# Attention, routed experts and an MLP on one core: the MLP takes the tokens in the order of their experts, and its first weights are prepared among the experts

## What is computed

```python
skip_score = x @ w_skip
do_compute = skip_score > 0
xc = x[do_compute]
logits = xc @ w_gate
e_idx = np.argmax(logits, axis=1)
for e in range(E):                       # 8 experts, hidden size 1024
    mask = e_idx == e
    h = np.maximum(xc[mask] @ w1[e], 0.0)
    y[mask] = gate_w[mask, None] * (h @ w2[e])
out[do_compute] = xc + y                 # the other tokens pass unchanged
...
h = x @ w_in                             # 512 -> 2048
g = h * np.clip(h + 3.0, 0.0, 6.0) / 6.0
return g @ w_out                         # 2048 -> 512
```

## Time and profile before

| | us |
|---|---|
| median of 3 runs (687.64 to 688.62) | 687.93 |
| the profiled execution's own time | 686.13 |
| its span | 684.5 |
| TensorE busy | 643.4 (94%) |
| VectorE busy | 397.9 (58%) |
| ScalarE busy | 323.6 (47%) |
| GpSimd busy | 71.6 (10%) |
| experts, from the first y to the last | 142 to 278.5 |
| MLP, from its first product | 290.4 to 681.2 |

### The profile page before, as it was taken

The page is one execution under the profiler, slowest core; times in us unless marked ns, Lnnn a source line. Parts: engine busy times, 40 slices in busy tenths (PEclk is TensorE's granted clock), DMA queues, the critical chain, the costliest instruction groups (busy, mean ns, idle before and its releaser), DMA issues.

```text
span 684.5 us, 17259 instructions
## 1 busy us (share of the span) xinstructions
PE 643.4 (94%) x6528; PEld 558.1 (82%) x6528; DVE 397.9 (58%) x1043; ACT 323.6 (47%) x675; POOL 71.6 (10%) x122
## 2 busy tenths in 40 slices
PE   5799986789999999989999999999999999999998
PEld 4678875667777887778889889898988988898986
DVE  2568875201111111568777767977777688777753
ACT  3689884011111111465544455655454566454433
POOL 4323452411111111000000000000000000000000
PEclk9999998789999999999999999999999999999999
DMA  9868869788587168632222221532222224212102
GB/s 169 168 161 195 197 180 385 234 304 313 191 274 274 31 216 271 204 101 63 77 78 78 61 71 54 200 118 93 82 63 62 62 68 148 63 61 63 32 0 93
DMA packets 118818, 95.10 MB, mean 139 GB/s; under 512 B 62737, under 2 KB 94485, under 8 KB 118752
## 3 DMA queue, kind: packets, MB, share of 16 engines
q1 hardware_dynamic: 103280, 61.79, 32.3%
q10 hardware_dynamic: 12496, 26.11, 11.2%
q0 software_dynamic: 2976, 6.32, 2.6%
HBM read 80.01 MB, written 17.52 MB: 142 GB/s over the span
## 4 chain that ended last, share of the span: by engine, by line
PE 80%; DMA 7%; DVE 6%; ACT 3%; issue 2%; SPq 1%; another core or an unknown queue 0%; POOLq 0%; POOL 0%; DVEq 0%; ACTq 0%
PE bank L1007 29%; PE av L956 25%; PE av L932 8%; PE bank L920 8%; DMA xin<-x_rows 5%; PE av L777 2%; PE bank L733 2%; DVE sm L1360 2%; PE bank L793 1%; PE bank L718 1%; PE av L889 1%; ACT pr L1054 1%; PE av L944 1%; DVE xall L1373 1%; DMA ot<-x_new 1%
## 5 line engine op out<-in xcount | busy, mean ns | idle before, releaser
L1007 PE MATMUL bank<-o_hi,g_lo 128*128 128x512 f32 x288 | 114.2, 397 | 0.0
L1007 PE MATMUL bank<-o_lo,g_hi 128*128 128x512 f32 x288 | 113.8, 395 | 0.0
L1007 PE MATMUL bank<-o_hi,g_hi 128*128 128x512 f32 x288 | 112.0, 389 | 0.0
L956 PE MATMUL av<-xc_hi,w_hi 128*128 128x384 f32 x342 | 89.1, 341 | 3.7 <-issue 1.9
L956 PE MATMUL av<-xc_hi,w_lo 128*128 128x384 f32 x342 | 87.7, 337 | 0.0
L956 PE MATMUL av<-xc_lo,w_hi 128*128 128x384 f32 x342 | 87.3, 336 | 0.0
L956 PEld LDWEIGHTS av<-xc_hi,w_hi 128*128 128x128 f32 x342 | 62.4, 188 | 19.3 <-DVE act L1615 3.6
L1622 DVE TENSOR_TENSOR g_lo<-act,g_hi 128x384 fp32r<-128x384 f32 x96 | 53.3, 555 | 40.2 <-ACT g_hi L1234 37.1
L920 PEld LDWEIGHTS bank<-xeT,w1s 128*64 128x64 f32 x2176 | 70.1, 140 | 6.5 <-issue 3.8
L920 PE MATMUL bank<-xeT,w1s 128*64 128x64 f32 x2176 | 72.3, 225 | 1.8 <-ACT xeT L1131 0.5
L1234 ACT CAST g_hi<-act 128x384 fp32r<-128x384 f32 x96 | 49.5, 516 | 50.9 <-DVE act L1615 50.9
(11 more groups left out here) (157 smaller groups left out, 910.2 us busy)
## 6 DMA issues: line engine op xcount, KB each, us to landing
w2s<-in_moe_w ACTq DMA_DIRECT2D x7, 2048.0 KB
wor<-in_moe_w_out SPq DMA_DIRECT2D x24, 512.0 KB, 3.7
w1s<-in_moe_w ACTq DMA_DIRECT2D x5, 2048.0 KB, 16.2
wir<-in_moe_w_in SPq DMA_DIRECT2D x24, 256.0 KB, 4.2
wir<-in_moe_w_in SPq DMA_DIRECT2D x48, 128.0 KB, 4.0
qraw<-in_q SPq DMA_DIRECT2D x36, 128.0 KB
vnow<-in_v SPq DMA_DIRECT2D x36, 128.0 KB
x_new<-xall SPq DMA_DIRECT2D x18, 256.0 KB
```

What stands on the lines that cost most here:

```text
L956: last = pe.matmul(into[:, 0:GN], a[it % 2][:, W_AT[w], c, :], b[:, X_AT[x], c, :], start=(n == 0 and fresh), stop=(n == 3 * XQ * len(pair ...
L1007: last = pe.matmul(bank[tile][:, :], a[c][:, i * P:(i + 1) * P], b[it % 2][:, units(it)[c], :], start=(plain(it) and c in (0, 2) and n == ...
```

## The change

The MLP no longer needs the tokens in their own order. `x_rows` gets a region of N + 64 rows ahead of the experts' regions. Skipping tokens count as a ninth class (`NC = NE + 1`), whose rows begin at 0 of that region: they are scattered straight to where the MLP reads them. The results of an expert tile are stored behind them as 64 consecutive rows with two direct DMAs (expert e begins at `first_row[e]`, in `rows_tbl`; rows beyond an expert's count are overwritten by the next expert). `x_new`, its 18 stores from the attention stage and the scatter by half rows are gone. The MLP reads 128 consecutive rows of 520 values; GpSimd copies their token numbers to `tok` (`take_tokens`) and scatters the results to the output by indirect DMA, 128 rows of 512 values each (`store_out`, 18 of them, on GpSimd instead of SP). SP waits before the first six tiles only for the `needed` expert tiles, those of experts that begin below row 768, and for all of them before it loads the second group.

The slices of the MLP's steps 0 and 1 are loaded by SP ahead of the rows of experts 2, 3, 4 and 5, and split by ScalarE behind the tiles of experts 3, 4 and 5 and by VectorE behind those of 3, 4 and 6. Tiles 3 to 5 of the first group get memory of their own (`x_first`). TensorE's spare matmuls between the experts and the MLP are removed.

```diff
+    R0 = N + ET
+    NC = NE + 1
...
-        xn = [put("X", f"xn{i}", [P, DM]) for i in range(3)]
+        xn = [put("X", f"xn{i}", [P, 2, HW]) for i in range(3)]
...
+        sums_at = at["X"]
         xd = [put("X", f"xd{i}", [P, XQ, GN]) for i in range(4)]
+        at["X"] = sums_at
+        x_first = [put("X", f"x_first{i}", [P, 2, HW]) for i in range(3)]
...
-        yo = sb("yo", [P, DH])
+        yo = sb("yo", [P, HW])
...
-        x_rows = nc.dram_tensor("x_rows", [(NE - 1) * R + TMAX * ET + ET, XW], fp32).ap()
-        x_new = nc.dram_tensor("x_new", [N, DM], fp32).ap()
+        x_rows = nc.dram_tensor("x_rows", [R0 + (NE - 1) * R + TMAX * ET + ET, XW], fp32).ap()
...
-            def store_x(T):
-                sp.wait_ge(s_x, T + 1)
-                sp.dma_start(x_new[T * P:(T + 1) * P, :].rearrange("s (h c) -> s h c", h=2), xall[:, T, :, 0:DH]).then_inc(s_xst, 16)
-
...
-            for T in range(1, NT + STORE):
+            for T in range(1, NT):
                 for n in loads_of(T):
                     load_qk(n)
-                if T < NT:
-                    load_v(T)
-                if T >= STORE:
-                    store_x(T - STORE)
-                if T == NT - 1:
-                    load_w1(sp, 0, s_wp1[0])
-                    load_w2(sp, 0, s_wp2[0])
-                    load_w1(sp, 1, s_wp1[1])
+                load_v(T)
+            load_w1(sp, 0, s_wp1[0])
+            load_w2(sp, 0, s_wp2[0])
+            load_w1(sp, 1, s_wp1[1])
...
+            for e, first, end in expert_tiles(sp, first_bounds(sp)):
...
+                elif e == 2:
+                    load_w_in(0)
+                elif e == 3:
+                    load_w_out(0)
+                elif e == 4:
+                    load_w_in(1)
+                elif e == 5:
+                    load_w_out(1)
+                with sp.Fori(0, end - first) as t:
+                    g = first + t
+                    row = t * ET + (R0 + e * R)
+                    sp.wait_ge(s_xet, g + XT0)
+                    sp.wait_ge(s_xmid, g + XM0)
+                    load_rows(bass.ds(row, ET))
+
...
+            total = end
+            sp.wait_ge(s_first, 1)
+            needed = sp.value_load(rows_tbl[0:1, NE:NC], min_val=0, max_val=TMAX)
+            sp.wait_ge(s_xet, total + XT0)
+            sp.wait_ge(s_xmid, total + XM0)
+            load_rows(slice(R0, R0 + ET))
+
...
-                sp.dma_start(x_tile(G, i)[:, :], x_new[T * P:(T + 1) * P, :]).then_inc(x_loaded(G, i)[0], 16)
...
-
-            for it in range(2):
-                load_w_in(it)
-                load_w_out(it)
-            sp.wait_ge(s_xst, 16 * NT)
-            sp.wait_ge(s_yst, total * 16 + YS0)
+                    sp.wait_ge(s_tok, T - 2)
+                sp.dma_start(x_tile(G, i)[:, :, :].rearrange("p h c -> p (h c)"), x_rows[T * P:(T + 1) * P, :]).then_inc(x_loaded(G, i)[0], 16)
+
+            sp.wait_ge(s_yst, needed * 32 + YS0)
...
+                if it == 0:
+                    sp.wait_ge(s_yst, total * 32 + YS0)
...
-            pool.wait_ge(s_xst, 16 * NT)
...
+            pool.wait_ge(s_first, 1)
             for e, first, end in expert_tiles(pool, bounds):
+                base = pool.value_load(rows_tbl[0:1, e:e + 1], min_val=0, max_val=N)
                 with pool.Fori(0, end - first) as t:
+                    row = t * ET + base
                     pool.wait_ge(s_yc, first + t + 1 + YC0)
                     fixed(pool)
-                    pool.indirect_dma_start(out=x_new.rearrange("n (h c) -> (n h) c", h=2),
-                                            out_offset=bass.IndirectOffsetOnAxis(ap=ytok[:, :], axis=0),
-                                            in_=yo[:, :], in_offset=None, bounds_check=2 * N - 1, oob_is_err=False).then_inc(s_yst, 16)
+                    for h in range(2):
+                        pool.dma_start(x_rows[bass.ds(row, ET), h * HW:(h + 1) * HW], yo[h * ET:(h + 1) * ET, :]).then_inc(s_yst, 16)
...
+            def take_tokens(G, i):
+                T = G * MT + i
+                pool.wait_ge(*x_loaded(G, i))
+                pool.tensor_copy(tok[:, T:T + 1], x_tile(G, i)[:, 0, TOKEN:TOKEN + 1]).then_inc(s_tok, 1)
+
+            def store_out(G, i, rows, signal):
+                T = G * MT + i
+                pool.wait_ge(s_tok, T + 1)
+                pool.indirect_dma_start(out=out, out_offset=bass.IndirectOffsetOnAxis(ap=tok[:, T:T + 1], axis=0),
+                                        in_=rows, in_offset=None, bounds_check=N - 1, oob_is_err=False).then_inc(signal, 16)
...
+            for G in range(MG - 1):
+                if G + 2 < MG:
+                    for i in range(3):
+                        take_tokens(G + 2, i)
+                for i in range(MT):
+                    pool.wait_ge(s_oca, MT * G + i + 1)
+                    store_out(G, i, ot[i % 3][:, :], s_ost[i % 3])
...
+            for i in range(3):
+                pool.wait_ge(s_oca, MT * MG - MT + i + 1)
+                store_out(MG - 1, i, ot[i][:, :], s_ost[i])
+            for i in range(3, 5):
+                pool.wait_ge(s_ocd, i - 2)
+                store_out(MG - 1, i, last_out(i), s_last)
+            pool.wait_ge(s_oca, MT * MG - MT + 4)
+            store_out(MG - 1, 5, last_out(5), s_last)
...
-            idle_turns(4)
-            total = tile_bound(pe, NE)
-            pe.wait_ge(s_xetc, total + 1)
-            fixed(pe)
-            idle_turns(3)
             for i in range(MT):
                 transpose_tile(0, i)
+            pe.wait_ge(s_xetc, end + 1)
+            pe.wait_ge(s_yc, end + YC0)
+            fixed(pe)
...
+                if e == 3:
+                    w_high(0)
+                    w_rest_high(0)
+                elif e == 4:
+                    o_high(0)
+                elif e == 5:
+                    w_high(1)
+                    w_rest_high(1)
...
-                sc.copy(xn[i - 3][:, cols], bank[i][:, cols]).then_inc(s_oca, 1)
...
-            total = sc.value_load(tbl[0:1, NE:NE + 1], min_val=1, max_val=TMAX)
-            sc.wait_ge(s_y, total)
-            fixed(sc)
-            w_high(0)
-            w_rest_high(0)
-            w_high(1)
-            w_rest_high(1)
-            o_high(0)
+                sc.wait_ge(s_tok, NT)
+                sc.copy(last_out(i)[:, cols], bank[i][:, cols]).then_inc(s_oca, 1)
...
-            take_last(5, slice(0, DH))
-            take_last(5, slice(DH, DM))
-            sc.wait_ge(s_oca, MT * MG - MT + 5)
-            sc.dma_start(out[N - P:N, DH:DM], xn[2][:, DH:DM]).then_inc(s_last, 16)
+            take_last(5, slice(0, DM))
...
+                then(dve.tensor_scalar(oh[:, 0:GT, NE:NC], skip, 0.0, 0.0, ALU.is_gt, ALU.is_equal))
...
-                then(dve.tensor_scalar(pskip[:, :], skip.rearrange("p t a -> p (t a)"), 0.0, float(NE * R), ALU.is_le, ALU.mult))
...
-                dve.tensor_tensor(pos[:, cols], psel[:, :], pskip[:, :], ALU.add).then_inc(s_pos, 1)
+                dve.tensor_copy(pos[:, cols], psel[:, :]).then_inc(s_pos, 1)
...
+            then(dve.tensor_tensor_scan(routed[:, :], one8[:, :], cnt[:, 0:NE], 0.0, ALU.mult, ALU.add))
+            then(dve.scalar_tensor_tensor(out=first_row[:, 0:NE], in0=routed[:, :], scalar=cnt[:, NE:NC], in1=cnt[:, 0:NE],
+                                          op0=ALU.add, op1=ALU.subtract))
+            then(dve.scalar_tensor_tensor(out=early[:, :], in0=first_row[:, 0:NE], scalar=float(MT * P), in1=ntl1[:, :],
+                                          op0=ALU.is_lt, op1=ALU.mult))
+            then(dve.tensor_reduce(first_row[:, NE:NC], early[:, :], axis=AX.X, op=ALU.add))
+            dve.tensor_copy(rows_tbl[:, :], first_row[:, :]).then_inc(s_first, 1)
...
-                    dve.wait_ge(s_yst, g * 16 + YS0)
-                    dve.tensor_copy(ytok[:, :], xres[:, TOKEN:TOKEN + 1])
+                    dve.wait_ge(s_yst, g * 32 + YS0)
+                    dve.tensor_copy(yo[:, DH:HW], xres[:, DH:HW])
                     dve.wait_ge(s_y, g + 1)
...
+                if e == 3:
+                    w_low(0)
+                elif e == 4:
+                    combine_w(1)
+                    o_low(0)
+                elif e == 6:
+                    w_low(1)
...
+                if G == 0:
+                    dve.wait_ge(s_tok, MT)
```

211 lines of the change are left out of this document (95 added, 116 removed).

## The result

The change made the kernel slower: 694.76 us (median of 5, 693.23 to 698.71) against 687.64 for 5 runs of before, ratio 1.0113 [1.0087, 1.0139]; on another chip 1.0170 [1.0146, 1.0193]. The time lies outside the range forecast (681.0 to 690.0), above it, where a small gain had been forecast. The profiled execution of the changed kernel is the slowest of its five, 698.71, and its span is 697.1.

A forecast was written before the change was run, and what follows sets the result against it. TensorE was taken to bound experts and MLP, with 11.9 us between last y and first product as the seam. Terms -8.0 + 4.4 + 0.8 + 0.2 + 0 = -2.6 us gave a median of 685.3, range 681.0 to 690.0.

The forecast's parts named there:

- The seam, -8.0: Between the experts' last y and the first MLP product: tiles loaded early, first product at 282.4 instead of 290.39, -8.0 us.
- the splits left in place: At the seam: weight splits not moved among the experts would delay the first product until 285.9, by 3.5 us.
- The end, +4.4: Last stores: GpSimd issues six scatters one behind the other, span ends at 688.9 against 684.5, +4.4 us.
- and 0.4 for the end as before: End of the kernel: from the last scatter's landing at 688.5 to the span's end, 0.4 us, giving 688.9.
- its upper bound of +6.4: End of the kernel: +6.4 us at the most, if each scatter's issue takes 1.30 us instead of 0.97.
- GpSimd's token copies at the seam: Seam: six copies of token numbers, due about 6 us after the first product, GpSimd free near 281; cost nothing.
- The experts, +0.8: Expert tiles: weights in SP's queue, results' stores and VectorE's splits move in; between 0 and +10, taken as +0.8 us.
- rival C: Experts: row loads of experts 2 to 5 stuck behind new weights in SP's queue; +10 us, 694.5; chance 0.15.
- Routing and attention, +0.2 and 0 (-2 to +1): Before the experts: ninth class on the chain +0.2 us; added rows against removed stores 0, bounds -2 and +1.
- the sign that it is wrong altogether: Attention, up to the first row load at 130 us: a move of more than 2 us means the prediction fails.
- B: End: six scatters don't queue, one's latency remains, +1.5 or less instead of +4.4; 682.4 or 681.4; chance 0.22.
- the Trainium skill's latency rule: End: first byte about 1 us for GpSimd's DMAs, 600 ns for SP's and ScalarE's; end +0.4 us, sum 681.3.

The follow-up runs named there:

- e4: e1 with the first two steps' weights loaded behind the last row load and split behind the last expert: 693.56 us, ratio 1.0065.
- e6: Kernel before with only the first two MLP steps' weights loaded and split early, among the experts: 683.60 us, ratio 1.0016.
- e12: e10 with the buffer addresses of e9, plus a ScalarE copy that waits for all result scatters: span ended at 681.0 us.
- e7: Changed kernel with SP storing all results directly, GpSimd only waiting for the last copy of results: 679.01 us, ratio 0.9941.
- e14: e10 with the buffer addresses of e9, and the wait for the scatters' completion moved from GpSimd to SP: 681.47 us, ratio 0.9994.
- e1: Changed kernel with GpSimd scattering results 0 to 2 ahead of the token copies at the group border: 690.94 us, ratio 1.0028.
- e10: e1 with a fourth result buffer, the last step's products reordered and the first weights one expert later: 683.50 us, ratio 1.0029.
- e9: e1 with the x tiles placed behind the buffers of g, p1, sums and hq: 686.77 us, ratio 1.0069.
- e2: Changed kernel with all results stored directly by SP, row after row, output not in token order: 678.20 us, ratio 0.9826.
- e13: Changed kernel with SP storing all results directly, plus one plain GpSimd DMA behind the last copy: 681.85 us, ratio 1.0000.
- r3: Kernel before, run again unchanged for a profile on a later chip: 682.32 us.
- e5: Kernel before with skipping tokens also scattered to rows of their own, and nothing else: 688.90 us, ratio 1.0077.
- e3: Kernel before with only its last six result stores made by GpSimd as scatters: 695.45 us, ratio 1.0089.
- r2: e2 run again on another chip: 676.52 us, ratio 0.9930.

## Why the prediction was wrong

**The seam, -8.0:** right, -9.4. The tiles lay ready, and the transposes of a tile take 0.5 us instead of 0.66. The prediction priced the splits left in place at 3.5 us (`e4`: 3.9); that they give next to nothing when they alone are moved (`e6`: 0.3) it did not say.

**The end, +4.4:** the first of two steps that failed. Its first terms hold to a tenth: the first scatter 0.8 us behind its copy, six of them 1.28 apart, landing in 2.8. The step "and 0.4 for the end as before" is wrong: `e12` has 6.6 us there, and 6.20 of them are GpSimd's DRAIN, which `e7` and `e14` move with the end of GpSimd's program. Before, SP's and ScalarE's queues did the last work, and the DRAIN, at 279.9, stood beneath the MLP: a cost that was hidden 400 us ahead of the end, in a row that the profile of before has. Measured, the term is +10.4, 6.0 more than forecast and beyond its upper bound of +6.4.

**The first border, not in the sum:** +6.3, the second step that failed. The prediction costed GpSimd's token copies at the seam and called them nothing; the same copies ahead of the first group's scatters, each waiting for a load that SP issues only then, it did not follow. It is what the rule "name what is queued behind the waiting instruction" asks for. `e1` gives back 4.6 of it, with the stretch at half the clock, and `e10` with a fourth buffer nearly all.

**The steady MLP, not in the sum:** +0.07 us a step, 1.7 us in all, from buffers that moved (`e9`).

**The experts, +0.8:** measured +0.9, but that proves little. Two versions with the same code up to the end of the experts, on one chip, take 145.9 and 142.2 us (`e1`, `e2`). The mechanism of rival C was there once (9.81 us for a row load), at a quarter of its price or less, and not in every execution. Eleven profiles have the weights at these places in SP's queue. Four have one such row load in the chain (9.3 to 9.8 us: the changed kernel, `e1`, `e6`, `e13`), seven have none over 7.6, and those with the weights elsewhere none over 7.9. So the missing row load of `e4` proves nothing about its edit. Why it comes at some times and not at others is open. The Trainium skill's rule of ring order (DMA: Bandwidth & Descriptors, Queues, rings and completion order) agrees with the slow row load, and the other seven profiles show that the order alone doesn't make one.

**Routing and attention, +0.2 and 0 (-2 to +1):** measured +2.6, of which 0.9 from the first to the last tile of attention, 0.7 from there to the last scatter, 0.8 from that to the first transposes. On the later chips the last two are +0.2 to +0.6 and -0.9 to +0.1: about the terms forecast. The first stays, some +1.0 (92.6 us in the mean of 11 profiles with the change in the routing, which reach from 91.2 to 93.8, and 91.6 in `r3`). Its cause is open; `e5`, with the added rows alone, has 92.2. The first row load moved from 129.66 to 132.71, by more than the 2 us that the prediction had named as the sign that it is wrong altogether. Some 2 us of such a shift can be the start of the program alone: the first tile of attention is ready at 19.1 to 19.5 us in some executions and at 21.0 to 21.5 in others, with the same code up to there, though these two profiles have 19.2 and 19.3.

**Rivals.** None of the five was it. That the time came out at C's 694.5 is chance: the loads that C stands on were stuck once and not four times, and the loss lay at the border and at the end. B, that the scatters don't queue, falls with the spacing of 1.28 us; the Trainium skill's latency rule, named beside it (Advanced Engine Details and Errata, DMA Advanced Topics), prices neither the queueing nor the 6.6 us behind the landing.

## What to carry to other kernels

Ask of each engine when it would end its last work, and what lies behind that: moving the last stores to an engine whose program used to end 400 us sooner cost 10 us here, more than half of it behind the landing of all data. Look for instructions that the busy time doesn't count, as a DRAIN at the end of a program: off the critical path they are free, and a change can put them on it. When two preparations lie over the same stretch, price the seam with each of them gone and with both. When an engine gets stores to issue, write down everything that it waits for ahead of each of them, at every repetition of the pattern, not at the first alone.

## What was not expected of the hardware

GpSimd closes its program with a DRAIN of 3.83 to 6.20 us, 0.08 us for each DMA that it has issued (46 to 75), and the span ends 0.23 us behind it (`e3`, `e7`, `e8`, the changed kernel). With GpSimd done long before, it is 2.6 us from the last copy to the end, the store included (`r2`). One form of matmul of 512 columns takes 395 ns or 389 ns by where in a partition its buffers lie (the changed kernel, `e9`). And writing 1412 more rows among the token scatters cost 5.3 us on one chip, where SP took 15.87 us instead of 12.44 to issue five stores beside them (`e5`, `r3`).
